# A chunked delta-rule attention with one 32x32 substitution in place of two 16x16 ones, and fewer, wider products

## The reference, cut to what matters

```python
def _attn_ref(q, k, v, beta):              # (4, 8, 768, 48) each, beta (4, 8, 768)
    k_n = k / (np.linalg.norm(k, axis=-1, keepdims=True) + 1e-06)
    state = zeros((B, H, D, D)); y = zeros_like(q)
    for t in range(S):
        kt, vt, bt = k_n[:, :, t], v[:, :, t], beta[:, :, t, None]
        y[:, :, t] = einsum('bhd,bhde->bhe', q[:, :, t], state)
        v_old = einsum('bhde,bhd->bhe', state, kt)
        state = state + bt[..., None] * einsum('bhd,bhe->bhde', kt, vt - v_old)
    return y

def reference(**kwargs):
    x = _attn_ref(...).transpose(0, 2, 1, 3).reshape(3072, 384)
    x = _moe_ref(x, ...)                   # top-1 of 8 experts, 384 -> 1024 -> 384
    return _moe2_ref(x, ...)               # RMS norm, gated MLP 384 -> 1536 -> 384
```

## Time and profile before

| | before |
|---|---|
| median of 3 runs | 1116.88 us (1113.96 to 1118.16) |
| profiled execution, its own time | 1122.8 us |
| its span | 1121.0 us |
| instructions of PE, DVE, ACT, POOL | 14266 MATMUL and as many LDWEIGHTS, 803, 607, 129 |
| busy PE, DVE, ACT, POOL | 950.7, 450.3, 340.2, 115.5 us |

### The profile page before, as it was taken

How to read it: one execution, slowest core, us unless ns; L and a number is a source line. 1 busy time by engine, 2 the same in 40 slices (tenths; PEclk the granted TensorE clock), 3 DMA queues, 4 the chain that set the end, 5 groups by cost and what they waited for, 6 DMA issues and landing times. The chain is left out here.

```text
span 1121.0 us, 31689 instructions
## 1 busy us (share of the span) xinstructions
PE 950.7 (85%) x14266; PEld 870.9 (78%) x14266; DVE 450.3 (40%) x803; ACT 340.2 (30%) x607; POOL 115.5 (10%) x129
## 2 busy tenths in 40 slices
PE   2373888888989994289999379999999999999997
PEld 2363787788888884289999368888888888888886
DVE  4445556463341124446666244432322323322222
ACT  3130232232213121145555254423223213232211
POOL 4110202020100000222433200000000000000000
PEclk9999997555555565679999779999999999999999
DMA  9403033311221003377666410020010200100101
GB/s 210 107 3 87 4 88 88 89 60 61 60 60 59 33 31 142 148 284 249 214 223 217 136 33 1 1 57 1 8 50 1 56 0 0 28 0 0 29 1 28
DMA packets 26739, 82.50 MB, mean 74 GB/s; under 512 B 4320, under 2 KB 16736, under 8 KB 23936
## 3 DMA queue, kind: packets, MB, share of 16 engines
q1 hardware_dynamic: 24192, 73.26, 21.3%
q0 software_dynamic: 2432, 7.47, 2.2%
HBM read 63.42 MB, written 17.30 MB: 72 GB/s over the span
## 5 line engine op out<-in xcount | busy, mean ns | idle before, releaser
L1358 PE MATMUL pg<-xT,wg 128*128 128x512 f32 x648 | 165.0, 398 | 1.7 <-DVE xT L1290 1.7
L1342 PE MATMUL po<-wo,hh 128*128 128x384 f32 x864 | 163.7, 337 | 0.1
L1358 PE MATMUL pv<-xT,wv 128*128 128x512 f32 x648 | 159.2, 390 | 0.0
L1342 PEld LDWEIGHTS po<-wo,hh 128*128 128x128 f32 x864 | 153.2, 188 | 5.6 <-DVE hh L1302 0.4
L1358 PEld LDWEIGHTS pv<-xT,wv 128*128 128x128 f32 x648 | 122.2, 189 | 26.3
L1358 PEld LDWEIGHTS pg<-xT,wg 128*128 128x128 f32 x648 | 121.1, 190 | 26.4 <-DVE xT L1290 3.0
L1300 DVE TENSOR_TENSOR hf<-pv,sil 128x512 f32<-128x512 f32 x72 | 49.8, 691 | 227.5 <-PE pv L1358 200.9
L1249 ACT CAST hh<-hf 128x512 fp32r<-128x512 f32 x72 | 44.7, 621 | 152.3 <-DVE hf L1300 152.3
L1245 ACT ACTIVATE sil<-pg 128x512 f32<-128x512 f32 x72 | 43.2, 600 | 151.0 <-PE pg L1358 150.9
L1092 PE MATMUL ph<-xh,w1h 128*128 128x256 f32 x576 | 72.8, 289 | 2.1 <-DVE xh L1041 2.1
L1092 PEld LDWEIGHTS ph<-xh,w1h 128*128 128x128 f32 x576 | 72.4, 198 | 2.5 <-issue 2.5
(11 more groups left out here) (191 smaller groups left out, 1319.8 us busy)
## 6 DMA issues: line engine op xcount, KB each, us to landing
w1s<-in_w SPq DMA_DIRECT2D x9, 1536.0 KB, 7.2
w2s<-in_w SPq DMA_DIRECT2D x9, 1536.0 KB
kT<-in_kT SPq DMA_DIRECT2D x24, 192.0 KB, 5.6
ktok<-in_ktok SPq DMA_DIRECT2D x12, 384.0 KB, 7.6
qT<-in_qT SPq DMA_DIRECT2D x24, 192.0 KB, 3.6
vt<-in_vtok SPq DMA_DIRECT2D x12, 384.0 KB, 4.7
x_gather<-xs SPq DMA_DIRECT2D x24, 192.0 KB, 3.3
x_next<-xs SPq DMA_DIRECT2D x24, 192.0 KB, 4.2
```

The lines of the kernel that those rows point to most:

```text
L1342: ins = nc.tensor.matmul(po[j][:, 0:DM], a[:, j * 128:(j + 1) * 128], w[:, f, :], start=(f == 0 and n == 0), stop=(f == K2 - 1 and n == 2))
L1358: ins = nc.tensor.matmul(ps[:], a[:, k, c], x[:, k, :], start=(k == 0 and n == 0), stop=(k == KD - 1 and n == 2))
```

## The change

One function and its inputs are written anew. Keys and queries come as one array `kq`, 128 partitions with each half padded from 48 to 64 rows; one product of a unit with 128 moving columns gives both k k^T and k q^T (`gram(g)`, in halves of 8 units), and one DVE operation masks both into `QA`. DVE substitutes whole 32x32 blocks in 30 steps, so `merge1`, `merge2` and `merge_out` go away; what was `blocks_zx` becomes `z_part` and `x_part`, at two places of the chunk. The values enter on TensorE as a product with a negated identity (`minus`) that is accumulated with k St in `pY`; ACT copies R and U out of PSUM (DVE did this with arithmetic), since -beta/|k|^2 is multiplied into the keys by POOL (`keys`). POOL's operations wait for `s_quiet`, which DVE raises ahead of `gram_out` and of the stream transposes. Grams are made 5 chunks ahead, at two places of a chunk.

```diff
-KRING, GRING, QRING = 8, 6, 3
-LEAD = 6
-SHARE = (3.0, 1.2, 1.3, 0.5)
+KRING, TRING, PRING = 6, 3, 4
+SHARE = (7.5, 4.5, 6.4)
...
 # DVE
-            def gram_out(c):
...
-                for p in range(2):
-                    v.tensor_tensor(units(p, Q[:, c % GRING]), bank(gram_banks(c)[p], C), units(p, MB[:, c % 2]),
-                                    ALU.mult).then_inc(s_q, 1)
+            def gram_out(c, a, signal=False):
...
+                v.tensor_tensor(QA[:, c % KRING, u], gram_bank(g)[:].rearrange("p two (i q n) -> p (two i) q n", q=2, n=C),
+                                MB[:, c % 2, u][:, :, None, :].broadcast_to([128, 8, 2, C]), ALU.mult).then_inc(s_q, 1)
...
-                for i in range(1, 15):
-                    w = 15 - i
+                for i in range(1, BLK - 1):
+                    w = BLK - 1 - i
+                    t = tmp[:, 0:i * w].rearrange("p (w k) -> p w k", k=i)
+                    link(v.tensor_tensor(t, W[:, i + 1:BLK, i:i + 1].broadcast_to([128, w, i]),
+                                         W[:, i:i + 1, 0:i].broadcast_to([128, w, i]), ALU.mult))
+                    link(v.tensor_tensor(W[:, i + 1:BLK, 0:i], W[:, i + 1:BLK, 0:i], t, ALU.add))
...
             for c in range(NC):
+                if c + 4 < NC:
+                    gram_out(c + 4, 1, True)
+                if c % 2:
+                    advance(work, 1000.0)
+                    if c // 2 + 1 < NC // 2:
+                        finish(c // 2 + 1, True)
+                    work = steps((c + 3) // 2, True) if c + 3 < NC else iter(())
+                advance(work, SHARE[c % 2])
+                if c + 5 < NC:
+                    gram_out(c + 5, 0, True)
+                advance(work, SHARE[2] if c % 2 else 1000.0)
+                if c in NORM_AT:
+                    norm(NORM_AT[c], True)
...
 # PE, per chunk
+                for p in range(2):
+                    ins = nc.tensor.matmul(pieces(pY[:, p, 0:DM]), minus[:],
+                                           vt[:, sv].rearrange("p (a two i) d -> p two a (i d)", two=2, i=4)[:, p],
+                                           start=True, stop=False, skip_group_check=True)
+                ins.then_inc(s_v, 1)
+                x_part(c)
...
+                pe.wait_ge(s_p, c + 1)
+                pe.wait_ge(s_q, min(2 * c + 10, 2 * NC))
...
 # ACT, per chunk
+                act.wait_ge(s_rf, c + 1)
+                for p in range(2):
+                    nc.scalar.copy(R[:, :, p], pieces(pY[:, p, 0:DM])).then_inc(s_r, 1)
+                x_out(c)
...
+                for p in range(2):
+                    act.wait_ge(s_uf, 2 * c + p + 1)
+                    nc.scalar.copy(U[:, :, p], pieces(pB[:, p, 0:DM])).then_inc(s_u, 1)
```

More of the change, by code:

```diff
@@ L143, in high, with parity, tokens, place @@
             return slice(t * HALF + BLK, t * HALF + 2 * BLK)
[L145 to L153, removed]
+        def parity(u):
+            return u // 4 % 2
+        def tokens(u, e):
+            return half(e ^ parity(u))
+        def place(u):
+            i = u // 8 * 4 + u % 4
+            return slice(i * D, i * D + D)
@@ L155, in _, with own, pieces, gram_bank @@
+        def own(x, rows, u):
+            return x[rows, u // 8, parity(u), u % 4 * D:u % 4 * D + D]
+        def pieces(bank):
+            return bank.rearrange("p (a x) -> p a x", a=2)
+        def gram_bank(g):
+            return pY if g < 6 and g % 2 else pB
         @block.sync
         def _(sp):
-            def load_k(c):
+            def load_kq(c, part):
                 s = c % KRING
-                for e in range(2):
-                    sp.dma_start(kT[half(e, D), s], kT_d[c, e]).then_inc(s_ld[s], 16)
-                sp.dma_start(ktok[:, s], ktok_d[c]).then_inc(s_ld[s], 16)
@@ L176, in _ @@
[L176 to L181, removed]
[L182 to L192 removed]
+                u = slice(part * 8, part * 8 + 8)
@@ new lines, in _ @@
+            load_kn(0)
+            sp.dma_start(beta[:], beta_d).then_inc(s_beta, 16)
+            for part in range(2):
+                load_kq(0, part)
+            for part in range(2):
+                load_kq(1, part)
+            sp.wait_ge(s_sq, 2)
+            load_kn(1)
+            load_vt(0)
+            load_kt(0)
+            sp.dma_start(wr[:], wroute_d).then_inc(s_wr, 16)
+            sp.wait_ge(s_q, 2)
+            for part in range(2):
+                load_kq(2, part)
+            load_vt(1)
@@ L447, in _ @@
             norm(0)
-            gram_out(0)
-            gram_out(1)
-            advance(invert(0), 1000.0)
+            for c in range(2):
+                for a in range(2):
+                    gram_out(c, a)
+            advance(steps(0), 1000.0)
+            finish(0)
             norm(1)
-            merge_out(0)
-            gram_out(2)
-            merge_out(1)
-            gram_out(3)
+            for c in range(2, 4):
+                for a in range(2):
+                    gram_out(c, a)
@@ L512, in merge1, with gram @@
-            def merge1(c):
-                s = c % GRING
-                w = BLK // 2
+            order = [8 * a + 4 * p + i for a in range(2) for i in range(4) for p in range(2)]
+            def gram(g):
+                c, a = divmod(g, 2)
+                s = c % KRING
+                pe.wait_ge(s_kq[s], 32 * (c // KRING + 1))
+                if g >= 2:
+                    pe.wait_ge(s_q, g - 1 if g < 6 else g)
+                bank = gram_bank(g)
+                for u in order[8 * a:8 * a + 8]:
+                    for e in range(2):
+                        ins = nc.tensor.matmul(bank[tokens(u, e), parity(u), u % 4 * 2 * C:u % 4 * 2 * C + 2 * C],
+                                               kq[half(e), s, u, 0:C], kq[half(e), s, u], start=True, stop=True)
+                ins.then_inc(s_gf, 1)
@@ L525, in merge1, with x_part @@
-                ins.then_inc(s_m1, 1)
-            def merge2(c):
-                s = c % KRING
-                w = BLK // 2
-                pe.wait_ge(s_m1e, c + 1)
+                    for t in range(2):
+                        ins = nc.tensor.matmul(pzx[high(t), u * BLK:u * BLK + BLK], QA[low(t), c % KRING, u, 0, BLK:C],
+                                               T[low(t), c % 2 * NP + u], start=True, stop=True)
+                ins.then_inc(s_zf, 1)
+            def x_part(c):
+                pe.wait_ge(s_ze, c + 1)
+                pe.wait_ge(s_p, c)
```

549 lines of the change are left out of this document (251 added, 298 removed).

## The result

The changed kernel takes 985.67 us (median of 4 runs, 979.96 to 993.75) against 1116.34 before: ratio 0.8836, 95% interval 0.8763 to 0.8909.

A forecast was written before the change was run, and what follows sets the result against it. TensorE bounds the attention, except in the first chunks, where it and DVE wait for each other. First chunks -36, middle -69, last -32: 1122.8 - 137 = 986, less 5.9 is 980, stated as 982; range 962 to 1050.

The forecast's parts named there:

- The clock, the open term: TensorE in the attention: denser products raise the clock in nearly every chunk; high level 60% of the time, bounds 0 and 100%.
- the forecast: The main case: TensorE's clock at the high level for over half of the time, 965 to 1015 us, chance 0.62.
- The products' prices: TensorE, low level, per chunk: values' product 2.8 us, each half gram 1.75, z_part and x_part 1.9 each; sum 26.9.
- The middle: the step that failed: Chunks 2 to 8: DVE is the bound, P R waits for gram_out; 114 us for 183.4, -69.
- The first chunks: Ahead of chunk 2: P R of chunk 1 starts at 104 after gram_out(5, 1), chunk 2 at 116 instead of 151.99, -36.
- The last chunks: From chunk 8: TensorE's alone, 90 / 1.6 = 56, plus 8 for turns and logits and 3 of waits: 67 for 99.1, -32.
- The waits: TensorE in the last chunks: 3 us of waits within the 67 predicted there.
- The transfers: Loads grow from 1.57 to 2.36 MB a chunk and stay hidden, also in a chunk of 18 us.
- POOL's stalls: In-between rival (chance 0.15 in all, 1015 to 1040): POOL stalls DVE steps, 33 us in middle and first chunks.
- The four squares: Slower rival, TensorE: the squares no longer work at once, +8.6 us a chunk, run at 1150 us; chance 0.03.
- ACT's copies of R: Sign of being wrong altogether: ACT's R or U copies come late by a microsecond or more each chunk.

The follow-up runs named there:

- e10: The changed kernel itself, unaltered, run again with more rounds: 985.76 us, 0.8839 of the kernel before.
- e1: The kernel before, with six more unused dense products ahead of each of the two transposes of a chunk: 1138.22 us, 1.0188 of before.
- e7: The changed kernel with three more unused dense products ahead of each transpose group: 993.41 us, 0.8895 of the kernel before.
- e8: The changed kernel with each wide gram product cut into two of 64 moving columns: 1008.08 us, 0.9027 of the kernel before.
- e2: The changed kernel with the values' product cut into two 64x64 squares, using half of the array: 997.47 us, 0.8917 of the kernel before.
- e3: The changed kernel with two more unused DVE reductions in each chunk, 5 us a pair of chunks: 1004.87 us, 0.8962 of the kernel before.
- e4: The changed kernel with POOL's operations no longer waiting for s_quiet: 991.43 us, 0.8855 of the kernel before.

## Why the prediction was right, and where it was not

It said 982 us, and the median is 985.67. For the profiled execution it had 986, and 993.75 was measured: the first chunks took 1.4 us less than predicted, the middle 4.8 more and the last chunks 5.6 more. That the median came within 4 us is partly luck: the profiled execution lies 8.1 above it, where 5.9 had been taken from the kernel before, and the middle of the same program took 7.7 us less in e10, twice the distance between forecast and result.

- **The clock, the open term.** Right in kind: what was called the forecast, over half of the time at the high level, is what happened, 70% in the middle (0.85) against the 60% chosen, 62% in the last chunks. That the clock moves the time is shown by e10 (7.7 us in the middle for 0.85 against 0.95), that dense products raise it by e1 and e7, and that the wide grams help to carry it by e8 (10 us in the middle at 0.78 instead of 0.85, of some 21 in all); e2 shows as much for the full-array product, by 9 to 12 us and a lower clock of the whole run. By the relation above the changed middle at the 0.53 of before would take 163 / (1 + 0.76 x 0.06) = 156 us of TensorE and some 12 of idle, 168: an estimate by which 50 of the 64.6 us come from the clock and 15 from less work and fewer waits. The Trainium skill (TensorE: Matmul & The Clock Gate, Part 1, What's actually happening) says that activity releases the throttled clock. Taken as busy time this does not decide between the kernels here: e8 is as busy as the changed kernel (90 and 89%) at 0.78 and 0.85.
- **The products' prices.** The values' product came at 2.84 us a chunk at the low level (2.8 taken), a half gram at 1.88 with 1.75 taken, `x_part` at 1.85 with 1.9; their sum over the middle is 6 x 26.9 - 1.75 = 160, and the relation gives 163 (an estimate).
- **The middle: the step that failed.** "DVE is the bound, because P R of a chunk waits for `gram_out`" is wrong: there is no such wait in the changed kernel, DVE is busy 96.80 of 118.78 us (81%, not the 90 that were named as a sign), TensorE 106.29. The 114 us were 108 of DVE and 6 for the clock; measured are 106 of TensorE and 12.5 of idle. The pauses that nothing in the profile releases were taken as 0.7 a chunk and are 1.7. DVE's own work was sized well (steps of 0.41 us at 240 elements, `gram_out` 1.22), and e3 shows how near it is. So the middle's time came out near for another reason than the one given: two engines with almost the same load.
- **The first chunks.** 116 for chunk 2's start, 114.6 measured, and P R of chunk 1 at 104 (104.12). But what the prediction has P R wait for, `gram_out(5, 1)`, ended at 101.0; what held P R was q St, which the working had not waiting at all:

```profile
97.99 0.23 ACT L330 ACTIVATE nrm<-n 128x32 f32<-128x32 f32 x1 [13.64 <-DVE n L435]
98.25 0.86 ACT L383 COPY R<-pY 128x384 f32<-128x384 f32 x2
```

ACT's queue stood at `root(3)` (L330) for 13.64 us until DVE came to `norm(3)`, and R's copies stood behind it. The prediction named what waits behind each DVE operation and not what waits behind ACT's.
- **The last chunks.** 67 predicted, 72.6 measured, and the share of the high level was right (0.62, 0.6 taken). The term that is off is the "90 / 1.6 = 56": it takes the high level to be twice as fast, and by rows 2 and the products above the factor is 1.76, so that 90 / (1 + 0.76 x 0.6) = 62. The waits were 6.1 us (72.58 - 66.46) instead of 3. The two together are more than the difference.
- **The transfers** were put at 2.36 MB a chunk and are 2.23 (two of 512 KB for `kq`, three of 384 KB). They stayed hidden: in the middle TensorE waits for none.
- **The rivals.** POOL's stalls, priced at 33 us if the cover failed, are worth 2 to 6 with no cover at all (e4). The four squares work at once as before: 26 to 28 ns a wide record at the high level. ACT's copies of R come 1.1 us late once in the middle, not by the microsecond or more in each chunk that was named as a sign of being wrong altogether.

## What to carry to other kernels

A TensorE stage of many small float32 products can be nine tenths busy and still at half its clock, as this one was (149.5 of 163.5 us at 0.50). Before removing products, look at the granted clock and at the duration of one repeated product. At equal time, try the form that fills more of the array or moves more columns per product; here both forms were the faster ones. An in-order engine that has been given a copy on the critical chain must be read whole: what stands ahead of the copy, and whom that waits for. And a kernel whose clock changes between its executions has a spread of its own (here 1.5% between runs), in which gains of 5 us on other engines can't be seen.

## What the runs showed that was not expected

- Cutting a product in two at no cost in TensorE's time (1.95 us a half gram in both forms at the low level, 1.1 at the high one) cost 2.1% of the whole run (e8); in the middle, where 10 us of it lie, the work is the same and the clock is lower.
- Products without use lengthened the kernel before by 21 us where their own time at the low level is some 61 (288 records of 0.21 us), and shortened the last chunks of the changed kernel by 3.6 us (e7).
- The profile's clock column says 1.00 before the first recorded rise (at 177 us before the change), while the products there take low-level times. A mean of the column over that stretch is too high; what is shown of the clock there is what the durations show.
